# Fewer array rows for the attention products of a fused attention and two-stage MLP kernel

## What is computed

```python
for t in range(S):
    kt, vt, bt = (k_n[:, :, t], v[:, :, t], beta[:, :, t, None])
    y[:, :, t] = np.einsum('bhd,bhde->bhe', q[:, :, t], state)
    v_old = np.einsum('bhde,bhd->bhe', state, kt)
    state = state + bt[:, :, :, None] * np.einsum('bhd,bhe->bhde', kt, vt - v_old)
...
h = np.maximum(x @ w_in, 0.0)                     # first MLP: 384 -> 2048 -> 384
x = h * h @ w_out
...
h = np.maximum(np.maximum(x @ w1, x @ w2), x @ w3)  # second MLP: 384 -> 3 x 768 -> 384
out = h @ w_out
```

## Time and profile before

| | |
|---|---|
| device time, median of 3 runs | 954.7 us (950.68 to 955.0) |
| profiled execution, its own time | 955.97 us |
| span of its trace | 954.0 us |
| PE busy | 875.1 us, 92% |
| PEld busy | 748.8 us, 78% |
| DVE, ACT, POOL busy | 436.3, 266.4, 287.6 us |

### The profile page before, as it was taken

One profiled execution on the slowest core, in us unless ns is written; L12 is line 12 of the kernel. 1 busy time (PEld: TensorE's weight loads), 2 busy tenths in 40 slices (PEclk: granted clock), 3 DMA queues, 4 the chain that ended last, 5 costly groups with the idle time before them and its releaser, 6 DMA issues.

```text
span 954.0 us, 20904 instructions
## 1 busy us (share of the span) xinstructions
PE 875.1 (92%) x9148; PEld 748.8 (78%) x9148; DVE 436.3 (46%) x639; ACT 266.4 (28%) x464; POOL 287.6 (30%) x394
## 2 busy tenths in 40 slices
PE   4107699989999999999999999999999999999998
PEld 4107578868888888878888888887898989898988
DVE  8683444664646464646543544434323232323231
ACT  2212144233223322332233223533222212122221
POOL 5427956951970196019600000632000000000000
PEclk9557799999999999999999999999999999999999
DMA  9964573337313731372142214112010202020000
GB/s 207 198 171 113 113 159 87 96 95 165 96 44 91 160 96 44 93 158 63 41 102 63 63 46 122 58 49 67 1 67 1 67 1 67 0 67 1 34 1 34
DMA packets 123435, 76.27 MB, mean 80 GB/s; under 512 B 94320, under 2 KB 107120, under 8 KB 123344
## 3 DMA queue, kind: packets, MB, share of 16 engines
q1 hardware_dynamic: 121088, 73.89, 31.9%
q10 hardware_dynamic: 2256, 1.05, 0.4%
HBM read 53.18 MB, written 20.45 MB: 77 GB/s over the span
## 4 chain that ended last, share of the span: by engine, by line
PE 89%; issue 4%; SPq 3%; DVE 2%; DMA 1%; ACT 1%
PE psum L71 25%; PE psum L72 24%; PE psum L73 24%; PE psum L595 3%; PE psum L671 3%; PE psum L659 2%; PE psum L620 2%; PE psum L609 2%; PE psum L646 2%; PE psum L635 2%; PE psum L678 2%; SPq L331 1%; SPq L326 1%; DMA kz<-in_kT 1%; DVE x_lo L963 0%
## 5 line engine op out<-in xcount | busy, mean ns | idle before, releaser
L974 DVE TENSOR_TENSOR sq<-relu 128x512 f32<-128x512 f32 x96 | 74.5, 776 | 155.6 <-ACT relu L1110 155.4
L71 PE MATMUL psum<-x_hi,win 128*128 128x512 f32 x288 | 116.9, 406 | 10.1 <-DVE x_lo L963 9.0
L73 PE MATMUL psum<-x_lo,wb 128*128 128x512 f32 x324 | 126.1, 389 | 0.0
L72 PE MATMUL psum<-x_hi,wb 128*128 128x512 f32 x324 | 126.1, 389 | 0.0
L71 PE MATMUL psum<-x_hi,wb 128*128 128x512 f32 x324 | 126.0, 389 | 0.0
L1110 ACT ACTIVATE relu<-psum 128x512 f32<-128x512 f32 x96 | 57.4, 598 | 231.7 <-PE psum L73 231.7
L71 PE MATMUL psum<-sq_hi,wout 128*128 128x512 f32 x288 | 114.0, 396 | 1.0 <-DVE sq_lo L979 1.0
L104 POOL TENSOR_TENSOR sol_tmp<-sol_b,sol_f 128x31 f32<-128x31 f32 (+15 forms) x155 | 91.9, 593 | 73.1 <-DMA sol_b<-dram_b 61.2
L72 PE MATMUL psum<-x_hi,win 128*128 128x512 f32 x288 | 113.5, 394 | 0.0
L73 PE MATMUL psum<-x_lo,win 128*128 128x512 f32 x288 | 113.4, 394 | 0.0
L72 PE MATMUL psum<-sq_hi,wout 128*128 128x512 f32 x288 | 112.1, 389 | 0.1
(11 more groups left out here) (99 smaller groups left out, 1304.3 us busy)
## 6 DMA issues: line engine op xcount, KB each, us to landing
kz<-in_kT SPq DMA_DIRECT2D x40, 192.0 KB, 3.6
qa<-in_qT SPq DMA_DIRECT2D x24, 192.0 KB, 3.9
v_t<-in_vn SPq DMA_DIRECT2D x12, 384.0 KB, 3.5
nz<-in_kn SPq DMA_DIRECT2D x24, 192.0 KB, 4.3
x2T<-x SPq DMA_DIRECT2D x6, 768.0 KB, 3.8
x_raw<-x2T SPq DMA_DIRECT2D x6, 768.0 KB, 4.6
out_dram<-o_t SPq DMA_DIRECT2D x24, 192.0 KB, 1.9
raw_wb<-in_w SPq DMA_DIRECT2D x18, 192.0 KB, 4.2
```

Source lines behind the costliest of these rows:

```text
L71: nc.tensor.matmul(out, lhs_hi, rhs_hi, start=first, stop=False)
L72: nc.tensor.matmul(out, lhs_lo, rhs_hi, start=False, stop=False)
L73: return nc.tensor.matmul(out, lhs_hi, rhs_lo, start=False, stop=last)
L974: nc.vector.tensor_tensor(d.sq[:], d.relu[:], d.relu[:], ALU.mult).then_inc(s.sq_ready, 1)
```

## The change

Seven of the eight products take slices of their operands: instead of all 128 partitions, only the 64 (or, in `x_block` and `g_block`, the 32) on which their own head's data lie. What was multiplied by zero is not read any more. The product `y` stays as it was, since it sums over both halves (state on one, update on the other). Tiles, loads, zeroing, outputs, waits and the order of the instructions on every engine are the same in both kernels. `half(h)` is the slice of partitions from 64h to 64h+63, `half(h, HALF)` that from 64h to 64h+31.

```diff
 def kk(c, b0):
-    last = nc.tensor.matmul(square_out(b0, p, h), kz[:, h, p, :], kz[:, h, p, :], start=True, stop=True)
+    last = nc.tensor.matmul(square_out(b0, p, h), kz[half(h), h, p, :], kz[half(h), h, p, :], start=True, stop=True)
 def qk(c, b0):
-    last = nc.tensor.matmul(square_out(b0, p, 1 - h), d.kz[:, h, p, :], d.qa[:, h, p, :], start=True, stop=True)
+    last = nc.tensor.matmul(square_out(b0, p, 1 - h), d.kz[half(h), h, p, :], d.qa[half(h), h, p, :], start=True, stop=True)
 def k_s(c):
-    last = nc.tensor.matmul(thin_out(6, p, h), d.kz[:, h, p, :], sw_of(h, p), start=True, stop=True)
+    last = nc.tensor.matmul(thin_out(6, p, h), d.kz[half(h), h, p, :], sw_of(h, p)[half(h)], start=True, stop=True)
 def x_block(c, b):
-    last = nc.tensor.matmul(bank[64 * h + HALF:64 * h + 64, b, p * HALF:(p + 1) * HALF], d.ob[:, p, :], d.f1[:, h, p, :],
+    last = nc.tensor.matmul(bank[64 * h + HALF:64 * h + 64, b, p * HALF:(p + 1) * HALF], d.ob[half(h, HALF), p, :], d.f1[half(h, HALF), h, p, :],
 def g_block(c, b):
-    last = nc.tensor.matmul(bank[64 * h:64 * h + HALF, b, p * HALF:(p + 1) * HALF], d.xt[:, p, :], d.fz[:, h, p, HALF:CH],
+    last = nc.tensor.matmul(bank[64 * h:64 * h + HALF, b, p * HALF:(p + 1) * HALF], d.xt[64 * h + HALF:64 * h + 64, p, :], d.fz[64 * h + HALF:64 * h + 64, h, p, HALF:CH],
 def f_d(c):
-    last = nc.tensor.matmul(thin_out(4, p, 1 - h), d.fz[:, h, p, :], d.d_t[:, p * HD:(p + 1) * HD], start=True, stop=True)
+    last = nc.tensor.matmul(thin_out(4, p, 1 - h), d.fz[half(h), h, p, :], d.d_t[half(h), p * HD:(p + 1) * HD], start=True, stop=True)
 def su(c):
-    last = nc.tensor.matmul(thin_out(4, p, h, HD), d.nz[:, h, p, :], sw_of(h, p), start=True, stop=True)
+    last = nc.tensor.matmul(thin_out(4, p, h, HD), d.nz[half(1 - h), h, p, :], sw_of(h, p)[half(1 - h)], start=True, stop=True)
```

## The result

The changed kernel takes 959.96 us (median of 5 runs, 958.79 to 963.19), the kernel before 954.7 us (median of 5, 950.68 to 958.72): ratio 1.0061, 95% interval 1.0041 to 1.0082. That is 5.3 us slower by the medians and some 5.8 us (3.9 to 7.8) by the ratio, which the text uses from here on. The profiled execution took 963.19 us (span 961.2), 3.2 us above its median; the one before, 955.97. Single traces of this kernel differ by several microseconds in where TensorE's clock falls and rises, so the time is split by the ratios of repeated runs, and the traces show places.

What follows compares the result with a forecast made beforehand. PE, busy 92% of the span, was taken to bound the kernel. 955.97 + 0 + 1.1 = 957.1 us, or 954.7 + 1.1 = 955.8 us on the median's scale; forecast alone 952 to 958, range with rivals 940 to 963.

Steps and rivals of the forecast that it cites:

- The dropped rows: In the seven narrowed products, batch time follows columns and heads already run two at a time: cost or gain 0.
- The step from `y` to `su`: New change of the array's division between these batches: 0.10 us each, 11 batches, + 1.1 us (0 to 2.2).
- Rival C: In the batches, two row groups cannot write one PSUM bank at once: 1050 to 1085 us, chance 0.07.
- A: In the batches, rows were the shared resource, so they get up to twice as fast: 890 us, chance 0.10.
- B: In the batches, only the fixed 8 ns per record pair shrinks: 938 us, or 947 for half, chance 0.09.
- Rival D: In the first stage, fewer working rows delay the clock: 5 to 8 us slower, 961 to 963 us, chance 0.08.
- Its sign: In the first stage, PEclk staying at 5 in the third to fifth slice, with batches at 3.7 us.

Runs made afterwards that it cites:

- mix_narrow: Changed kernel with `qk` issuing all first heads, then all second, and later `kk` interleaving pairs p and p + 8 with the latter's output halves swapped; 979.92 us.
- later_only: Changed kernel with narrow rows only behind the first stage, all 128 rows within it; 956.99 us, ratio 1.0043 to the kernel before.
- first_only: Changed kernel with narrow rows only in the first stage, 128 rows in every later batch; 956.74 us, ratio 1.0035 to the kernel before.
- xg_only: Kernel before with only `x_block` and `g_block` on 32 rows for each head; 957.45 us, ratio 1.0037 to the kernel before.
- the bursts: Kernel before with two bursts of constant-tile matmuls in PE's first-stage wait, on 128 rows (958.97 us) or on 32 then 64 rows (957.66 us).
- filler: Constant-tile matmuls on 128 rows added in PE's first-stage waits: ratio 0.9998 on the kernel before, 1.0048 on the changed kernel, both against the kernel before.

## Why the prediction was right or wrong

**The dropped rows, 0: right.** The batches kept their length (`kk` 2.01 us, `k_s` 2.00, `x_block` 1.13); only the single records of `x_block` became 5 ns shorter (median 191 against 196 ns). The reason held as well: two at a time by output half (3.73 us for `qk` without it). The Trainium skill (TensorEngine Tiling (Array Packing), Theoretical Speedup) names up to 2x; `mix_narrow` agrees (2.01 to 1.09 us), for four parts in turn, and this change leaves two.

**The step from `y` to `su`, + 1.1: right, the size by luck in part.** It is 0.10 us as taken from the step in columns, and 0.03 more at the end of `su`, which the prediction did not have: 9 x 0.13 = 1.2 us on the path. The prediction's sum took 11 batches, though it names 9 on the path.

**Rival C, one bank for two row groups: did not come.** By the Trainium skill (TensorEngine Tiling (Array Packing), Gotcha 1: PSUM Pressure) read literally `kk` would have slowed; at 2.01 us the trace disagrees, for row groups that write different partitions of a bank.

**Rivals A and B: out** as stated, with unchanged batches.

**Rival D, the clock: it came, and the forecast had put it aside.** The step of the working that failed is "Behind 115 us the MLP's matmuls, unchanged, hold the clock at 1.00; that attention batches of 2 to 4 us would drop it there is unlikely", and the chance of 0.08 with it. The profile of before shows that the clock was never below 1.00 there, not how near it was to falling. With `x_block` and `g_block` on 32 rows, the idle of 1.68 us that it used to get over is followed by a fall, which cost 1.6 us in the trace compared and 2.9 in that of `later_only`. D's reason (fewer rows count as less work) fits; its price for the first stage (5 to 8 us) was too high against the 3.3 measured for `first_only`. Its sign, 5 in the third to fifth slice of PEclk, came only in part: the row reads 5, 5, 8 there, with batches of 3.7 us up to 87 us, and 5, 7, 7 before.

The 5.8 us are then 1.2 for the step, 3.5 for the two 32-row products (`xg_only`, interval 1.7 to 5.3), and 1.1 left over, within the intervals. That the clock is how the two products cost time is shown for the fall near 425 us; for the rest of their 3.5 us, in the first stage, it is argued from the bursts and from the mean clock of the runs, since single profiles there differ by as much from run to run. The measured 960.0 us lies inside the range that D had widened, not inside the forecast's own 952 to 958: the total was covered by a rival with a chance of 0.08, and by no reasoning of the forecast. PE busy, forecast within 2 us of 875, came out at 878.5.

No version here beats the kernel before. Not tried: an order in which two different products with opposite halves (say `kk` and `f_d`) alternate. By what `mix_narrow` shows, that should give four parts in turn, with every result in its place.

## What to carry to other kernels

Dropping zero rows from a small matmul saves nothing by itself: count how many independent parts of the array the order of issue keeps in turn, since only that shortened a batch here. Check what else the rows were doing: here rows of zeros went with a clock that stayed up, and the one new change of the array's division cost 0.1 us each time. A clock that stands at full in every slice says nothing of its margin; look for idles inside dense stretches before thinning the work around them.

## What was not expected of the hardware

- Two float32 products of 32 columns on 32 rows each, 11.9 us with 1.04 us of idle, did not raise the clock; on 128 rows an unbroken 5.67 us did, and 4.45 us did not.
- Four 64x64 parts in turn gave 1.09 us a batch against 2.01.
- A clock that got over idles of 1.68 and 2.07 us in a dense stage with 128-row batches fell behind idles of 1.93 and 1.98 us in two other kernels with the same batches.
- PE pauses in the middle of a batch with nothing to wait for in the profile: 1.68 us at the same instruction in both kernels, and more of them with filler. In the bursts the stretches between them hold 128 or 256 records for the most part. What they are is open.
